# Turning the expert stage's operands as two halves of 64 rows into two banks

## What is computed

```python
def _moe2_ref(x, w_skip, w_gate, w1, w2):
    do_compute = x @ w_skip > 0
    out = x.copy()
    xc = x[do_compute]
    logits = xc @ w_gate
    e_idx = np.argmax(logits, axis=1)
    ...
    for e in range(E):
        mask = e_idx == e
        h = np.maximum(xc[mask] @ w1[e], 0.0)
        y[mask] = gate_w[mask, None] * (h @ w2[e])
    out[do_compute] = xc + y

def reference(**kwargs):
    attn_out = _attn_ref(**attn_kwargs)
    x = attn_out.transpose(0, 2, 1, 3).reshape(B * S, H * D)
    x = _moe_ref(x=x, **moe_kwargs)
    return _moe2_ref(x=x, **moe2_kwargs)
```

## Time and profile before

| | us |
|---|---|
| median of 3 runs | 791.35 (788.58 to 791.63) |
| profiled execution, its own time | 791.72 |
| its span | 789.9 |
| PE busy | 758.0 (96% of the span) |
| PEld busy | 639.8 (81%) |
| DVE busy | 524.1 (66%) |
| ACT busy | 347.8 (44%) |
| POOL busy | 245.3 (31%) |
| mean granted TensorE clock | 0.993 of full speed |

### The profile page before, as it was taken

One profiled execution on the slowest core, in us unless ns is written; L12 is line 12 of the kernel. 1 busy time (PEld: TensorE's weight loads), 2 busy tenths in 40 slices (PEclk: granted clock), 3 DMA queues, 4 the chain that ended last, 5 costly groups with the idle time before them and its releaser, 6 DMA issues.

```text
span 789.9 us, 15565 instructions
## 1 busy us (share of the span) xinstructions
PE 758.0 (96%) x5170; PEld 639.8 (81%) x5171; DVE 524.1 (66%) x1331; ACT 347.8 (44%) x830; POOL 245.3 (31%) x240
## 2 busy tenths in 40 slices
PE   5999999899999999999999999999987999999995
PEld 3777777688998888898988998888865777887884
DVE  3888888954337974984797598436665997367342
ACT  3888888644322213223222322324452774446231
POOL 4888887944501201210121021000112231222211
PEclk9999999999999999999999999999998999999998
DMA  9556677462422112101210200502424898174000
GB/s 163 133 149 157 163 162 188 144 198 61 147 79 103 48 57 91 50 21 62 59 41 0 90 22 27 214 0 81 135 95 126 270 340 303 46 229 153 34 15 9
DMA packets 101061, 88.15 MB, mean 112 GB/s; under 512 B 63812, under 2 KB 78532, under 8 KB 100880
## 3 DMA queue, kind: packets, MB, share of 16 engines
q1 hardware_dynamic: 95584, 81.89, 34.7%
q0 software_dynamic: 3056, 5.00, 1.9%
q10 hardware_dynamic: 2368, 0.59, 0.4%
HBM read 72.26 MB, written 18.34 MB: 115 GB/s over the span
## 4 chain that ended last, share of the span: by engine, by line
PE 86%; ACT 5%; DVE 4%; issue 3%; DVEq 1%; DMA 1%; POOL 0%; SPq 0%; ACTq 0%; POOLq 0%
PE h_ps L1733 12%; PE out_ps L1733 12%; PE h_ps L1734 12%; PE h_ps L1735 12%; PE out_ps L1735 11%; PE out_ps L1734 11%; PE o_ps L684 5%; PE s_ps L668 3%; ACT prob L541 3%; PE t_ps L593 2%; PE out_ps L1869 1%; PE s_ps L663 1%; ACT pt L525 1%; PE tr_ps L1834 1%; DMA raw_qk<-in_q_dram 1%
## 5 line engine op out<-in xcount | busy, mean ns | idle before, releaser
L1558 ACT ACTIVATE ex<-h_ps 128x384 f32<-128x384 f32 x96 | 47.3, 493 | 272.3 <-PE h_ps L1735 272.3
L1733 PE MATMUL h_ps<-xt_hi,wi_hi 128*128 128x384 f32 x384 | 131.8, 343 | 0.0
L1734 PE MATMUL h_ps<-xt_lo,wi_hi 128*128 128x384 f32 x384 | 129.7, 338 | 0.0
L1735 PE MATMUL h_ps<-xt_hi,wi_lo 128*128 128x384 f32 x384 | 129.7, 338 | 0.0
L1394 DVE TENSOR_SCALAR ex<-ex 128x384 f32<-128x384 f32 x96 | 36.9, 385 | 131.1 <-ACT ex L1558 129.7
L1733 PE MATMUL out_ps<-wo_hi,gt 128*128 128x512 f32 x288 | 114.5, 398 | 0.0
L1735 PE MATMUL out_ps<-wo_hi,gt 128*128 128x512 f32 x288 | 113.9, 396 | 0.0
L1734 PE MATMUL out_ps<-wo_lo,gt 128*128 128x512 f32 x288 | 113.3, 393 | 0.0
L541 ACT ACTIVATE prob<-s_ps,negmax 128x128 f32<-128x128 f32 (+2 forms) x144 | 77.8, 556 | 14.1 <-DVE negmax L399 13.7
L1276 DVE CUSTOM_DVE_ANT_0 x2t<-x,w_raw 128x512 bf16<-128x512 f32 x108 | 82.7, 806 | 0.4
L1172 POOL TENSOR_TENSOR xt_lo<-x_raw,xt_hi 128x384 fp32r<-128x384 f32 x20 | 28.3, 1413 | 157.8 <-ACT xt_hi L1575 157.5
(11 more groups left out here) (180 smaller groups left out, 1589.0 us busy)
## 6 DMA issues: line engine op xcount, KB each, us to landing
w_raw<-in_moe_w_dram SPq DMA_DIRECT2D x56, 512.0 KB, 5.2
raw_qk<-in_q_dram SPq DMA_DIRECT2D x32, 144.0 KB, 3.2
attn_t<-attn_sb SPq DMA_DIRECT2D x16, 288.0 KB, 2.2
x_raw<-attn_t SPq DMA_DIRECT2D x24, 192.0 KB, 2.4
w_raw<-recip_rows SPq DMA_DIRECT2D x48, 96.0 KB, 2.8
out_dram<-x SPq DMA_DIRECT2D x18, 256.0 KB, 2.1
x_rows<-x SPq DMA_DIRECT2D x18, 256.0 KB, 2.6
v<-in_v_dram SPq DMA_DIRECT2D x32, 128.0 KB, 2.9
```

The source lines that it names most:

```text
L1558: act.activation(ex[:, f % 2], h_ps[:, f % 2, 0:NB], ACT.Exp).then_inc(ex_done, 1)
L1733: pe.matmul(dst, stat[0], mov[0], start=start, stop=False, skip_group_check=True)
L1734: pe.matmul(dst, stat[0], mov[1], start=False, stop=False, skip_group_check=True)
L1735: return pe.matmul(dst, stat[1], mov[0], start=False, stop=stop, skip_group_check=True)
```

## The change

From the second tile on, a group of four turns of 128 x 128 becomes a group of eight turns of 64 rows: for each of the four blocks, rows 0 to 63 go to the first of two banks and rows 64 to 127 to the second. The result of `turn_x` then takes half of each of the banks of `tr_ps` and `lg_ps`, which become one tensor `tl_ps`; the result of `turn_h(t, j)` takes columns 256 j to 256 j + 255 of both banks 0 and 1 of `out_ps`. ACT and DVE read the same 512 values for each partition through a pattern over two banks (2 x 4 x 64). `hold` stands ahead of each group. `turn_h` waits for the low part of the turn just before it rather than the one before that, since both now use both banks.

```diff
-        tr_ps = ctx.enter_context(nc.psum_tensor("tr_ps", [P, BANK], F32))
-        lg_ps = ctx.enter_context(nc.psum_tensor("lg_ps", [P, BANK], F32))
+        tl_ps = ctx.enter_context(nc.psum_tensor("tl_ps", [P, 2, BANK], F32))
+        tr_ps, lg_ps = tl_ps[:, 0], tl_ps[:, 1]
...
+        HALF_P = P // 2
+        ROWS = [slice(h * HALF_P, (h + 1) * HALF_P) for h in range(2)]
+        def by_halves(banks, at):
+            return banks[:, :, at:at + KC * HALF_P].rearrange("p h (k t) -> p h k t", k=KC)
+        def xt_turned(t):
+            if is_zero(t):
+                return xt_bank(t).rearrange("p (k t) -> p k t", k=KC), lambda x: x
+            return by_halves(tl_ps, 0), lambda x: x.rearrange("p k (h t) -> p h k t", h=2)
+        def ht_turned(t, j):
+            if is_zero(t):
+                return ht_ps[:, j].rearrange("p (k t) -> p k t", k=KC), lambda x: x
+            return (by_halves(out_ps[:, 0:2], j * KC * HALF_P),
+                    lambda x: x.rearrange("p k (h t) -> p h k t", h=2))
...
-                act.activation(mxt[0][:, :, :], xt_bank(t).rearrange("p (k t) -> p k t", k=KC),
-                               ACT.Copy).then_inc(xt_hi_done, 1)
+                turned, as_turned = xt_turned(t)
+                act.activation(as_turned(mxt[0][:, :, :]), turned, ACT.Copy).then_inc(xt_hi_done, 1)
...
-                for k in range(KC):
-                    last = pe.transpose(xt_bank(t)[:, k * P:(k + 1) * P], x_now[:, k * P:(k + 1) * P],
-                                        ident[:, :])
+                if is_zero(t):
+                    for k in range(KC):
+                        last = pe.transpose(xt_bank(t)[:, k * P:(k + 1) * P], x_now[:, k * P:(k + 1) * P],
+                                            ident[:, :])
+                else:
+                    hold(pe, held_pe)
+                    for k in range(KC):
+                        for h2, rows in enumerate(ROWS):
+                            last = pe.transpose(tl_ps[:, h2, k * HALF_P:(k + 1) * HALF_P],
+                                                x_now[rows, k * P:(k + 1) * P], ident[rows, rows])
...
-                wait(pe, ht_lo_done, HALVES * (t - 1) + j + 1)
+                wait(pe, ht_lo_done, HALVES * (t - 1) + j + 1 if is_zero(t) else HALVES * t + j)
...
+                    hold(pe, held_pe)
+                    for k in range(j * KC, (j + 1) * KC):
+                        for h2, rows in enumerate(ROWS):
+                            last = pe.transpose(out_ps[:, h2, k * HALF_P:(k + 1) * HALF_P],
+                                                h[rows, k * P:(k + 1) * P], ident[rows, rows])
```

More of the change, by code:

```diff
@@ L960, in experts @@
         final_done = sem("final_done")
-        held = sem("held_f")
+        held, held_pe = sem("held_f"), sem("held_pe_f")
         def blocks(step):
@@ L1460, in xt_low @@
                 dve.wait_ge(xt_hi_done, t + 1)
-                dve.tensor_tensor(mxt[1][:, :, :], xt_bank(t).rearrange("p (k t) -> p k t", k=KC),
-                                  mxt[0][:, :, :].bitcast(F32), ALU.subtract).then_inc(xt_lo_done, 1)
+                turned, as_turned = xt_turned(t)
+                dve.tensor_tensor(as_turned(mxt[1][:, :, :]), turned, as_turned(mxt[0][:, :, :]).bitcast(F32),
+                                  ALU.subtract).then_inc(xt_lo_done, 1)
             def ht_low(t, j):
                 dve.wait_ge(ht_hi_done, HALVES * t + j + 1)
-                dve.tensor_tensor(ht[1][:, j * KC:(j + 1) * KC, :],
-                                  ht_ps[:, j].rearrange("p (k t) -> p k t", k=KC),
-                                  ht[0][:, j * KC:(j + 1) * KC, :].bitcast(F32),
+                turned, as_turned = ht_turned(t, j)
+                ks = slice(j * KC, (j + 1) * KC)
+                dve.tensor_tensor(as_turned(ht[1][:, ks, :]), turned, as_turned(ht[0][:, ks, :]).bitcast(F32),
                                   ALU.subtract).then_inc(ht_lo_done, 1)
@@ L1668, in ht_high @@
                     act.wait_ge(ym_done, t)
-                act.activation(ht[0][:, j * KC:(j + 1) * KC, :],
-                               ht_ps[:, j].rearrange("p (k t) -> p k t", k=KC),
+                turned, as_turned = ht_turned(t, j)
+                act.activation(as_turned(ht[0][:, j * KC:(j + 1) * KC, :]), turned,
                                ACT.Copy).then_inc(ht_hi_done, 1)
@@ L1865, in turn_h @@
             def turn_h(t, j):
-                wait(pe, ht_lo_done, HALVES * (t - 1) + j + 1)
+                wait(pe, ht_lo_done, HALVES * (t - 1) + j + 1 if is_zero(t) else HALVES * t + j)
                 pe.wait_ge(relu_done, HALVES * t + j + 1)
-                for k in range(KC):
-                    last = pe.transpose(ht_ps[:, j, k * P:(k + 1) * P],
-                                        h[:, (j * KC + k) * P:(j * KC + k + 1) * P], ident[:, :])
+                if is_zero(t):
+                    for k in range(KC):
+                        last = pe.transpose(ht_ps[:, j, k * P:(k + 1) * P],
+                                            h[:, (j * KC + k) * P:(j * KC + k + 1) * P], ident[:, :])
+                else:
+                    hold(pe, held_pe)
[3 more added lines that the diff above has]
+                                                h[rows, k * P:(k + 1) * P], ident[rows, rows])
                 last.then_inc(ht_done, 1)
```

## The result

| | before | after |
|---|---|---|
| median of 8 runs each, us | 791.76 (788.40 to 792.23) | 794.76 (792.98 to 797.11) |
| profiled execution, its own time | 791.72 | 794.31 |
| its span | 789.9 | 792.4 |

The ratio is 1.0051, with an interval from 1.0038 to 1.0064: the changed kernel is slower by 4.0 us (3.0 to 5.1). The table's medians differ by 3.0 us, the means of the eight runs by 3.8, so 4.0 is good to about one microsecond. The interval lies around the 0.5% bound itself.

The account below looks back on a forecast made before the run. PE, busy for 96% of the span, was taken to bound the kernel. At 0.16 us for each group, less slack, the tiles summed to +3.9 us: 795.3 us on the median 791.35, range 790.8 to 799.0.

Parts of the forecast that it names:

- Going in: Between the product ahead and the half turns: 0.27 us instead of 0.17 in attention, so +0.10 us a group.
- Eight halves and going out: From the first half turn to the next 128-row product: 0.39 us, made of 0.27 for turns and 0.12 going out.
- The product behind: First product behind the half turns takes 0.28 us instead of 0.17 in attention: +0.11 us; today's group pays 0.09.
- 0.16 us for a group: Each changed group on PE costs 0.60 us against 0.44, a loss of 0.16 us, bounds 0.12 to 0.20.
- `hold` at nothing: The semaphore instruction ahead of each group on PE's sequencer costs nothing, or up to 0.1 us where the sequencer is last.
- Slack, tiles 2 to 5: Losses of 1.76 us in these tiles against 1.7 us of waits that DVE sets: 0.1 us left.
- second rival: All 43 groups pay: no slack is used, 43 x 0.16 = 6.9 us, giving 798.3 us; chance 0.15.
- Slack, tiles 8 to 10: Three `turn_h` of second halves pay 0.48; six other groups' 0.96 meets 0.7 us of waits, leaving 0.26: together 0.74 us.
- Tile 14: 0.16, then 0.32 against 0.15 us of wait: 0.33 us; the last `turn_h` costs 0 as chunk 4 waits for it.
- Faster: Rival: changes of shape cost nothing beside 512-column products, a group costs 0.27 us, -3.6 us in all: 787.8; chance 0.1.
- The halves run in turn: Rival: the two halves run one after the other, 0.43 us for a group, about 806 us; chance 0.02.
- no difference: Rival: passages cost about what the turns save, within 0.05 us a group: 791.3 us, give or take 1; chance 0.08.

Follow-up runs that it names:

- 12 blocks: The kernel before with each group of turns of h issued three times, x once: in halves 806.77 us, whole 812.51 us.
- the extra passage: The changed kernel with, in each group, an 8-column product of 128 rows and another pair of half turns behind the eight: 807.03 us, 1.0214 on before.

## Why the prediction was right, step by step

- **Which time counts.** PE without idle time from 661 to 686 and 727 to 762 us meant that each group there is paid in full. It was: +0.92 us for six groups, +1.37 for nine, about 0.15 us each, 0.46 us a tile against the forecast's 0.48.
- **Going in, 0.10 us,** taken from attention's 0.27 against 0.17: 0.33 against 0.23. Right, and it belongs to the halves themselves, since `hold` alone leaves it at 0.23.
- **Eight halves and going out, 0.39 us**: 0.39. The prediction split it in 0.27 + 0.12. Start to start, the last half takes 0.152 us where one more in a row takes 0.031 on average, so what eight halves cost above their share of a long row is about 0.14 us. Right in size, but not all of it is going out: 0.05 us of it lies behind the first block of the group. Right too that two halves run side by side: they start 0 to 7 ns apart, and a block takes 0.0625 us against 0.109.
- **The product behind, +0.11 us:** 0.34 against 0.23. Right. Whole groups pay 0.09 for the same; it is no price of halves as such.
- **0.16 us for a group:** 0.152. The sum is high by about 0.2 us for this.
- **`hold` at nothing:** nothing, except where the sequencer is last. The "up to 0.1 us" for that was short: 0.08 to 0.18 us at tiles 4, 9 and 14, about 0.3 us in all in the kernel with `hold` alone. In the changed kernel it is there too: from the end of the copy of `x_now` to chunk 0 it takes 2.13, 1.92 and 1.89 us at these tiles, where it took 1.97, 1.80 and 1.72. In both kernels the sequencer's last instruction ends 0.06 us ahead of chunk 0 there, and DVE's `ht_lo` 0.2 us or more.
- **Slack, tiles 2 to 5:** forecast +0.1, measured +0.33. This term was mis-sized. I had set all 1.7 us of waits, as DVE's, against 1.76 us of losses. At tile 4 the gap from the last turn to chunk 0 is as long as it was, 0.44 us. The sequencer was last there and not DVE. It starts on its branches behind the copy of `x_now`, and it comes 0.16 us later behind that copy than in before, of which `hold` makes 0.14 (the kernel with `hold` alone):

```profile
646.34 0.46 PE L1862 MATMUL tl_ps<-ident_f,x_now 64*128 64x64 f32 x8
647.02 0.49 PE L1754 MATMUL out_ps<-wo_hi,ht_hi 128*128 128x512 f32 x1 [0.22 <-issue]
```

  In before the same wait was put down to DVE's `ht_lo`, which hid that the sequencer stood right behind it. And DVE's own chain came later along with PE, though it was busy for 95% of the stretch. Up to tile 3 its work stands where it stood (the copies of `x_now` are shifted by -1.07 us, as at tile 2). At tile 4 `final` waits for PE's last output chunk, and the copies come at -0.91, one group's loss later:

```profile
643.12 0.75 DVE L1476 SCALAR_TENSOR_TENSOR x2t<-out_ps,gw_past,x_past 128x512 f32<-128x512 f32 x1 [0.20 <-DVE gw_past L1472]
```

  In before that gap was 0.05 us. At tile 5 the copies come at -0.75. There PE's chunk 0 starts without a gap of its own and DVE's `ht_lo` ends 0.06 us ahead of it, so both are last, and these 0.32 us of DVE are the +0.33 of PE. So both mechanisms of the second rival were there, at tiles 4 and 5. The gaps at tiles 2, 3 and 5 shrank from 0.40, 0.59 and 0.46 us to 0.24, 0.29 and 0.15, of which 0.15 is now the bare passage.
- **Slack, tiles 8 to 10:** forecast 0.74, measured 0.60. The waits were used up more fully than thought: the gaps behind `turn_x` of 0.30, 0.27 and 0.30 us became 0.15, 0.24 and 0.15, so that only tile 9's, where the sequencer is last, is more than the bare passage.
- **Tile 14:** forecast 0.33, measured 0.33. Its wait behind `turn_x` shrank from 0.16 to 0.04 us, nearly as forecast, though it was the sequencer's and not DVE's, and chunk 4's wait took the last group. The counterpart of the earlier trace rows, where 0.51 us were 0.43 after, and the last wait of 0.43 is 0.21:

```profile
776.32 0.46 PE L1862 MATMUL tl_ps<-ident_f,x_now 64*128 64x64 f32 x8
776.75 0.50 PE L1754 MATMUL out_ps<-wo_hi,ht_hi 128*128 128x512 f32 x1
...
780.62 0.50 PE L1754 MATMUL out_ps<-wo_hi,ht_hi 128*128 128x512 f32 x1 [0.21 <-DVE ht_lo L1489]
```

- **What would show it.** The end of tile 5 moved by 0.33 us from the end of tile 1, under the 0.5 that was given. "The waits shrunk to nearly nothing" was right at tiles 5, 8, 10 and 14, half right at 2 and 3, and wrong at 4.
- **The rivals.** *Faster* fell with the first row of the halves: the product ahead takes 0.33 us and not 0.23, though it has 512 columns. *All 43 groups pay* (+6.9 us) fell with the gaps that shrank, though a part of it came true in tiles 4 and 5. *The halves run in turn* fell with 0.39 us for eight, and *no difference* with the interval from 1.0038.
- **How close it came.** The price of a group and the stretches without waits were right for the reasons given. That the sum meets the runs to 0.1 us is in part luck: in the table tiles 2 to 5 were forecast 0.23 us too low, tiles 8 to 10 0.14 too high and the others 0.16 too high, which nearly cancels, and the runs themselves say no more than 3.0 to 5.1 us.

The Trainium skill's page "TensorEngine Tiling (Array Packing)" bore on this from both sides. Its "Theoretical Speedup", up to two for a dimension of 64, came out as 0.109 / 0.0625 = 1.7 for the turns alone, at 12 blocks still as 1.23 / 0.90 = 1.4 from the group's start to the next product, and as a loss at four blocks. Its "Key Properties" say that a change of mode drains the engine. The trace agrees in that no weight load runs ahead across the change, and the extra passage in that each change has its price, which here decided the sign.

## What to carry to other kernels

Half-array turns in pairs are worth it where a row of them is long or, to judge by attention's rows, its neighbours use half arrays too: here a group pays 0.35 us once and saves 0.047 us for each block of 128 x 128, so four blocks lose and twelve win. Read such a cost from start to start, from the product ahead to the one behind, since the busy time of the turns falls while the kernel gets slower. And slack behind a branch is only slack if the engine's own sequencer, not the releaser that the view names, has time to spare; a long row of instructions in front of the branch takes that time. Nor is a busy engine's chain fixed: with DVE busy for 95% of a stretch, 0.32 us of PE's 1.7 still went through it.

## What the runs showed that I had not expected

- **The sequencer's lead can vanish at once.** With 12 half turns ahead of a branch its first instruction behind them ran 1.37 us ahead of the turns' start, with 16 it ran 0.02 us behind it, at 13 of 15 groups. Sixteen whole turns, also 32 instructions, kept 0.44 us. At four tiles with a load of the next expert's number the loss is 1.1 to 1.4 us each. Where between 24 and 32 instructions the bound lies, and why the two kernels differ, stays open.
- **No weight load is drawn ahead across a change of shape.** A whole group's first load starts 0.23 us ahead of its first turn, a half group's with it, at all 42 groups from `turn_h(1, 0)` on.
- **A product of 8 columns is about as dear a neighbour as one of 512:** 0.16 us out of the halves into it and 0.11 us back, its own time included.
- **The clock's slow stretch around tile 1 moves between executions** by 2 us or more, which is half of the effect measured here. Two spans alone would have given +2.5 us where the runs give +4.0.
